# A constant of one column moved from its own tile into the tile of the softmax sums

## The reference

```
scores = q @ k.T / sqrt(64)
keep = is_sink | (0 <= rel < window)
a = softmax(where(keep, scores, -1e9)); x = a @ v        # x: [1536, 512]

h = x @ w_in                       # layer 0
g = where(h >= 1, h, where(h <= -1, 0, (h + 1)**2 / 4))
x = g @ w_out

h = x @ w_in2                      # layer 1
g = where(h > 0, h, exp(min(h, 0)) - 1)
out = g @ w_out2
```

## Time and profile before

| | |
|---|---|
| median of 3 runs | 645.17 us (645.09 to 645.34) |
| the profiled execution | 645.09 us |
| its span, first to last instruction | 643.4 us |
| TensorE busy | 621.7 us, 97% |
| VectorE busy | 377.6 us, 59% |
| ScalarE busy | 349.7 us, 54% |
| GpSimd busy | 74.5 us, 12% |
| granted clock of TensorE | 1.00 |

### The profile page before, as it was taken

How to read it: one execution, slowest core, us unless ns; L and a number is a source line. 1 busy time by engine, 2 the same in 40 slices (tenths; PEclk the granted TensorE clock), 3 DMA queues, 4 the chain that set the end, 5 groups by cost and what they waited for, 6 DMA issues and landing times.

```text
span 643.4 us, 12200 instructions
## 1 busy us (share of the span) xinstructions
PE 621.7 (97%) x4164; PEld 555.4 (86%) x4164; DVE 377.6 (59%) x994; ACT 349.7 (54%) x830; POOL 74.5 (12%) x147
## 2 busy tenths in 40 slices
PE   5788999999999999999999999999999999999997
PEld 3678889999999999999999988888888888888886
DVE  6899968886886788588757863322332222322221
ACT  5777756666675676566656663333443333633333
POOL 5212212320321222123000000000000000000000
PEclk9999999999999999999999999999999999999999
DMA  8664212320322222022045500000100000100001
GB/s 283 222 209 133 88 41 66 105 66 25 103 66 62 64 71 86 35 81 90 21 164 164 188 10 0 1 0 1 50 17 0 0 0 0 65 0 0 0 0 65
DMA packets 15275, 42.48 MB, mean 66 GB/s; under 512 B 2852, under 2 KB 4536, under 8 KB 15248
## 3 DMA queue, kind: packets, MB, share of 16 engines
q0 software_dynamic: 7040, 20.57, 10.4%
q1 hardware_dynamic: 8208, 21.56, 9.7%
HBM read 38.98 MB, written 3.15 MB: 65 GB/s over the span
## 4 chain that ended last, share of the span: by engine, by line
PE 86%; DVE 10%; ACT 2%; issue 1%; DMA 0%; ACTq 0%; SPq 0%; DVEq 0%
PE h_ps L507 13%; PE h_ps L509 12%; PE h_ps L508 12%; PE y_ps L522 10%; PE y_ps L524 9%; PE y_ps L523 9%; PE s_ps L524 3%; PE s_ps L523 3%; PE s_ps L522 3%; PE o_ps L490 3%; PE t_ps L470 2%; DVE wout_lo L840 1%; PE s_ps L461 1%; PE s_ps L460 1%; DVE win_lo L840 1%
## 5 line engine op out<-in xcount | busy, mean ns | idle before, releaser
L507 PE MATMUL h_ps<-x_hi,win_hi 128*128 128x256 f32 (+1 forms) x576 | 184.8, 321 | 0.9 <-DVE g_full L866 0.6
L509 PE MATMUL h_ps<-x_hi,win_lo 128*128 128x256 f32 (+1 forms) x576 | 182.8, 317 | 0.0
L508 PE MATMUL h_ps<-x_lo,win_hi 128*128 128x256 f32 (+1 forms) x576 | 182.5, 317 | 0.0
L522 PE MATMUL y_ps<-g_hi,wout_hi 128*128 128x256 f32 (+1 forms) x480 | 145.6, 303 | 2.0 <-DVE g_lo L853 1.9
L524 PE MATMUL y_ps<-g_hi,wout_lo 128*128 128x256 f32 (+1 forms) x480 | 145.0, 302 | 0.0
L523 PE MATMUL y_ps<-g_lo,wout_hi 128*128 128x256 f32 (+1 forms) x480 | 144.9, 302 | 0.0
L870 DVE SCALAR_TENSOR_TENSOR g_full<-g_full,h_ps 128x512 f32<-128x512 f32 x48 | 33.0, 688 | 151.7 <-ACT g_full L675 151.7
L507 PEld LDWEIGHTS h_ps<-x_hi,win_hi 128*128 128x128 f32 x576 | 108.2, 188 | 10.3 <-DVE g_full L866 1.1
L508 PEld LDWEIGHTS h_ps<-x_lo,win_hi 128*128 128x128 f32 x576 | 108.1, 188 | 8.4
L509 PEld LDWEIGHTS h_ps<-x_hi,win_lo 128*128 128x128 f32 x576 | 108.2, 188 | 7.2
L662 ACT CAST g_hi<-g_full 128x256 fp32r<-128x256 f32 (+1 forms) x144 | 68.5, 476 | 69.7 <-DVE g_full L866 34.9
(11 more groups left out here) (109 smaller groups left out, 814.5 us busy)
## 6 DMA issues: line engine op xcount, KB each, us to landing
ks<-in_k POOLq DMA_DIRECT2D x40, 260.0 KB, 2.9
raw<-in_w_in SPq DMA_DIRECT2D x11, 512.0 KB, 4.3
raw<-in_w_out SPq DMA_DIRECT2D x11, 512.0 KB, 4.4
qs<-in_q POOLq DMA_DIRECT2D x40, 128.0 KB, 2.7
vals<-in_v POOLq DMA_DIRECT2D x20, 192.0 KB, 3.0
out_y<-xy SPq DMA_DIRECT2D x12, 256.0 KB, 2.1
xy<-in_w_in SPq DMA_DIRECT2D x5, 512.0 KB, 7.1
xy<-in_w_out SPq DMA_DIRECT2D x5, 512.0 KB, 4.2
```

The lines of the kernel that those rows point to most:

```text
L507: pe.matmul(o, win_hi[:, k, f], x_hi[:, k, :], start=(k == 0), stop=False)
L508: pe.matmul(o, win_hi[:, k, f], x_lo[:, k, :], start=False, stop=False)
L509: last = pe.matmul(o, win_lo[:, k, f], x_hi[:, k, :], start=False, stop=(k == KT - 1))
L522: pe.matmul(o, wout_hi[:, t, cols], g_hi[:, t % GR, :], start=begin, stop=False, skip_group_check=True)
```

## The change

The tile `half` goes. `small` is made twice as wide, 32 columns in place of 16, and `half` is now the name of its 17th column. The views `tops` and `totals` take the same 16 columns as before. The memset at L893 then fills one column in place of 64; the activations at L718 and L670 read the new column.

```diff
-        small = sb("small", [P, IN_FLIGHT * 4 * QB])
+        small = sb("small", [P, 2 * IN_FLIGHT * 4 * QB])
         tops, totals = (small[:, n:n + IN_FLIGHT * 2 * QB].rearrange("p (s h j) -> p s h j", s=IN_FLIGHT, h=2)
                         for n in (0, IN_FLIGHT * 2 * QB))
         top, total = tops[:, 0, :, :], totals[:, 0, :, :]
+        half = small[:, IN_FLIGHT * 4 * QB:IN_FLIGHT * 4 * QB + 1]
...
         ramp, g_full = sb0("ramp", [P, 2, CT]), sb0("g_full", [P, 2, CT])
-        half = sb0("half", [P, 64])
...
-            nc.scalar.activation(t_ps[:, 0:1], half[:, 0:1], ACT.Exp)
+            nc.scalar.activation(t_ps[:, 0:1], half[:, :], ACT.Exp)
```

## The result

The changed kernel takes 651.98 us (median of 6 runs, 650.91 to 654.30) against 645.23 for the kernel before (6 runs). The ratio is 1.0106, with a 95% interval of 1.0087 to 1.0126. The prediction was "the same", 644.0 to 646.3 us, and was wrong. In some executions of every kernel the granted clock was lower for a part of the first 88 us, which made them 1 to 3 us longer, and three executions among the experiments (767.36, 876.07 and 2,164.52 us) are left out of all medians and ratios. The shortest executions of the two kernels are 6.0 us apart, the profiled ones 5.8.

What follows compares the result with a forecast made beforehand. TensorE, busy 621.7 of 643.4 us, was taken to bound the kernel, except VectorE in the first 85 us. The profiled 645.09 us plus terms of 0 gave 645.1 us, range 644.0 to 646.3.

Steps and rivals of the forecast that it cites:

- What bounds the kernel: Whole kernel: TensorE bounds it, busy 621.7 of 643.4 us, except the first 85 us, which are VectorE's.
- (a): First of three ways a change could move the time: the pace of TensorE's matmuls.
- The constant itself: Memset at L893 writing 1 column for 64: at best 0.11 us shorter, covered by idle time, worth 0.
- the bias operand: 96 activations at L670 reading their bias from small: at most 0.4 us on ScalarE either way, taken as 0.
- VectorE and ScalarE: Their pace on moved tiles: four starts lie on one line within 2 ns; bound 0.3 us either way, taken as 0.
- The first transfer: First qs pieces on the start-up path, ahead of TensorE's first matmul at 3.60: 0 to 0.4 us saved, taken as 0.
- The fifth of 2.2 us: First qs transfer: qs rows might need four pieces instead of five from a 256-byte boundary, saving 0.4 us.
- TensorE: Matmuls of both layers streaming the moved tiles: other starts give the same pace, so 0.
- The witness: Scores' matmuls, 260 columns from starts 0, 32, 16, 48: 118.75 ns on average against 119.2 by the line.
- The start of a row can touch the fixed part alone: Layer matmuls, 0.435 ns a column plus 6.2 ns fixed: a tile's start could change only the 6.2 ns.
- Rival 2: Layer matmuls slower because a start at a multiple of 256 costs 2.5 ns each: 8.6 us, 653.7 us; chance 3%.
- Rival 1: Layer matmuls faster as the fixed 6.2 ns goes: all 21.4 us, likeliest half, 10.7 us, 634.4 us; chance 3%.

Runs made afterwards that it cites:

- f2_const_64: The changed kernel with small 320 bytes wide instead of 128, moved tiles at distance 64 from the weights as before the change; 645.67 us, ratio 1.0007.
- f4: The kernel before with 64 unused bytes ahead of the tiles of layer 1, only these at distance 128 from the weights; 650.2 us, ratio 1.0073.
- g1: The kernel before with 192 unused bytes ahead of layer 1's tiles, these at distance 0 from the weights, layer 0's at 64; 645.25 us, ratio 0.9977.
- e1: The kernel before with 64 unused bytes behind small, half untouched, moved tiles of both layers 64 bytes later; 651.01 us, ratio 1.0076.
- e2: The changed kernel with small 640 bytes wide instead of 128, moved tiles still at distance 128 from the weights; 650.98 us, ratio 1.0077.
- e4: The kernel before with 64 unused bytes ahead of the weights, so weights and moved tiles shift together, distance still 64; 647.08 us, ratio 1.0010.
- f3: The kernel before with 64 unused bytes behind small and 192 ahead of layer 1's tiles, only layer 0's at distance 128; 649.5 us, ratio 1.0062.
- m2_fine: No layer computed, TensorE alone: distances in 16-byte steps, shorter weight loads, other widths, odd matmuls ahead of blocks; best 226.7 ns (512 columns), 113.3 (256).
- m1_distance: No layer computed, TensorE alone: blocks of 36 matmuls at distances 0 to 992 bytes in steps of 32; 226.7 to 234.4 ns for 512 columns.
- e3_rem128: The kernel before with 192 unused bytes behind small, moved tiles at the weights' remainder, distance 0; 646.55 us, ratio 1.0004.

## Why the prediction was wrong

**What bounds the kernel** was read rightly: the loss is TensorE's pace, (a) in that list, and the traces show no other.

**The constant itself, the bias operand**: right, 0. L670 stayed at 474 ns, and f2_const_64 has the constant in `small` at no cost.

**VectorE and ScalarE**: right. L853 stayed at 692 ns, L782 went from 698 to 699. Their pace does not depend on where a tile starts, at the starts tried.

**The first transfer**: the first matmul ran at 3.42 us in place of 3.60, and the first maximum at 5.24 in place of 5.43. That lies between the two ends of 0 and 0.4 us, but the other traces don't put it down to where `qs` starts.

```profile
3.42 1.65 PE L427 MATMUL s_ps<-qs 64*128 64x128 f32 x8 [3.42 <-DMA qs<-in_qk_first]
```

In the four traces with `qs` at 192 modulo 256 (before, f2, f4, g1) the first matmul ran at 3.48 to 3.66 us, in the five at 0 (changed, e1, e2, e4, f3) at 3.42 to 3.62, and the first issue at 0.88 or 0.89 in all. The fifth of 2.2 us is not there. The Trainium skill, "DMA: Bandwidth & Descriptors", section "How a descriptor splits into AXI transactions", says that a transfer which starts off a multiple of 256 bytes fetches from the boundary below; these runs show no gain from starting on one. (Here the side that is written moved, and the rule speaks of what is fetched.)

**TensorE** is the step that failed: "So other starts give the same pace", and with it the term of 0. The new start gave 232.4 ns for 228.9 in layer 1 and 118.8 for 117.8 in layer 0, 5.9 us together. Three things were wrong in the step.

- The question was put for one address. Each matmul reads two tiles, and what counts is how far they lie apart. The prediction lists that the moved tiles go from 192 to 0 and that the weights keep their place, and never takes the difference, 64 to 128.
- The witness was the wrong one. The scores have weights of their own, `q_parts`, and their distances from those were 0, 16, 32 and 48 bytes; neither 64 nor 128 was among them. They have 260 columns, where TensorE alone took 119.4 to 120.8 ns in all four blocks, so they could hardly show anything. And they come in fours between other matmuls, while the rhythm of layer 1 is 3 matmuls long before the change and 7 after it.
- "The start of a row can touch the fixed part alone, since inside a row all is contiguous" made an upper bound out of a picture of how a row is read. The changes from distance to distance at 512 columns, up to 7.7 ns, exceed the whole fixed part of 6.2 ns. The split of the pace into 0.435 ns a column and 6.2 ns was itself an accident of distance 64. At distance 0 the same split gives (226.7 - 120.0) / 256 = 0.417 ns a column and 13.3 ns fixed; from the best pace of either width, 226.7 and 113.3, it would be 0.443 and 0.

Rival 2 had the right engine and the right sign, with 8.6 us where it was 6.8, and was given 3%. (Its price was half of what its own rows give: if only `k_hi` costs, a pair that is 5 ns longer is 5 ns on one matmul, not 2.5, and 17 us on 3,456. So its nearness to the result is luck.) Its mechanism, that a multiple of 256 costs, is refuted by e4_all_moved. Rival 1 named the gain: with another distance some 7 us do go, though not as a fixed cost at an edge. The Trainium skill, "TensorE: Matmul & The Clock Gate", section "Wait — 56ns, not 53.3ns?", gives the number of columns divided by 2.4 GHz plus 2.5 ns from start to start; an estimate by it is 109.2 and 215.8 ns for 256 and 512 columns. The least that any distance gave here is 113.3 and 226.7.

The range does not quite follow from its terms either: they add up to 643.8 to 646.1, not 644.0 to 646.3, which changes nothing here.

The chance was the deeper mistake. The one part that touched 97% of the span was answered by eight matmuls printed to 0.01 us, which bounds it to 1.25 ns or 4.3 us, and this bound was then left out of the range as a rival of 3%. And the trace held a hint, below the 0.01 us of a printed row. In layer 1 of the kernel before the distances from start to start repeat as 226, 229 and 232 ns, while all these matmuls have the same form and none waits. Such a rhythm says that more than the number of columns sets the pace, and that is a reason not to price a new layout at 0.

## What to carry to other kernels

When a kernel is bound by TensorE, treat the byte offset between the tile of the weights and the moved tile as a parameter like a tile's size, measured anew for each width of matmul and of weight load. Any edit that allocates, frees or resizes a tile between the two can move the whole kernel by a per cent without one instruction changed, and such an edit is compared at equal offsets, with unused bytes put in where needed. Distances from start to start that repeat in a pattern some ns wide (226, 229, 232) are a sign that the layout costs time; an even pace is no proof of the contrary, as the 233, 233, 234 ns at distance 192 show. An untouched neighbour is a witness for a cost only if it has the same width, the same partner and as long a run.

## What the runs showed of the hardware

- float32r matmuls of 128 by 128 weights, one load for each: 226.7 to 234.6 ns for 512 columns and 113.3 to 120.0 for 256 (the settled blocks of the runs of TensorE alone), by the distance between moved and weight tiles at multiples of 16 bytes, repeating every 256 bytes.
- A distance of 4 bytes from a multiple of 16 was worse than any other tried, 238.0 ns for 512 columns.
- At some distances the stream has more than one stable rhythm: 113.3 and 117.8 ns for 256 columns at distance 192 in m2_fine, 232.1 to 232.7 and 233.3 for 512 columns at distance 128 in m1_distance. In the kernel, at distance 64, the two of 256 columns made 1.3 us over a chunk of 384 matmuls. What decides between them is open.
- Shorter weight loads moved the pace both ways (m2_fine): 512 columns ran at 231.0 to 231.7 ns with loads of 32 columns, for 226.7 to 233.3 with 128, and 256 columns mostly faster, 113.3 ns at three of four distances. The mechanism stays open.
- In some executions the granted clock was lower for a part of the first 88 us. It was 0.95 in the stage from 20 to 88 us of the profiled e3_rem128, a mean between full speed (2.4 GHz) and half of it, and 1.00 there in the kernel before. What decides it was not tested.
